# Attention output turned by one fp32r matmul per block, with its halves split by GpSimd and its sums moved by DMA

## What is computed

```python
q_pool = q.reshape(B, H, S // 2, 2, D).mean(axis=3)          # B=2, H=8, S=1152, D=64
scores = scale * np.matmul(q_pool, k.transpose(0, 1, 3, 2))
attn = np.exp(scores - np.max(scores, axis=-1, keepdims=True))
attn = attn / (np.sum(attn, axis=-1, keepdims=True) + 1e-09)
x = np.matmul(attn, v)      # then heads side by side: 1152 rows of 512
logits = x @ w_gate
noise_scale = np.log1p(np.exp(x @ w_noise))                  # both: 512 x 8
noisy_logits = logits + noise_scale * noise                  # picks two experts per row
...
```

## Time and profile before

| | |
|---|---|
| median of 3 runs | 845.34 us (844.6 to 846.09) |
| the profiled execution | 844.89 us, span of its trace 843.1 us |
| TensorE busy | 831.5 us (99%) |
| VectorE, ScalarE, GpSimd busy | 510.8, 418.7, 401.5 us |
| attention stage | up to about 305 us, of it 12 cycles of 18.0 us in the loop |
| granted TensorE clock | 1.000 over the span |

### The profile page before, as it was taken

How to read it: one execution, slowest core, us unless ns; L and a number is a source line. 1 busy time by engine, 2 the same in 40 slices (tenths; PEclk the granted TensorE clock), 3 DMA queues, 4 the chain that set the end, 5 groups by cost and what they waited for, 6 DMA issues and landing times.

```text
span 843.1 us, 15376 instructions
## 1 busy us (share of the span) xinstructions
PE 831.5 (99%) x4860; PEld 743.2 (88%) x4861; DVE 510.8 (61%) x1003; ACT 418.7 (50%) x770; POOL 401.5 (48%) x293
## 2 busy tenths in 40 slices
PE   7999999999999999999999999999999999999998
PEld 6999999999999898888887888888888999999997
DVE  7888888888888886322322223232286875576554
ACT  4777777777777774211211111121145765565554
POOL 8654455546887005548969959577432020000000
PEclk9999999999999999999999999999999999999999
DMA  5212111142241016887645635353445021000101
GB/s 131 71 45 82 43 42 42 42 148 80 92 151 69 1 57 222 299 302 231 234 145 187 199 137 199 131 192 131 143 124 164 1 75 38 2 0 1 38 1 37
DMA packets 51520, 91.27 MB, mean 108 GB/s; under 512 B 9376, under 2 KB 18592, under 8 KB 50976
## 3 DMA queue, kind: packets, MB, share of 16 engines
q1 hardware_dynamic: 40832, 67.26, 24.0%
q10 hardware_dynamic: 7296, 12.59, 4.5%
q0 software_dynamic: 3360, 11.01, 4.5%
HBM read 73.78 MB, written 17.06 MB: 108 GB/s over the span
## 4 chain that ended last, share of the span: by engine, by line
PE 94%; POOL 2%; DVE 1%; DMA 1%; issue 1%; ACT 1%; ACTq 0%; POOLq 0%; DVEq 0%
PE ps L1729 10%; PE ps L1731 10%; PE ps L1730 10%; PE ps L1536 5%; PE ps L1573 5%; PE ps L1589 5%; PE ps L1591 4%; PE ps L1590 4%; PE ps L1574 4%; PE ps L1885 4%; PE ps L1884 4%; PE ps L1883 4%; PE ps L1845 4%; PE ps L1843 4%; PE ps L1844 4%; PE ps L1527 3%
## 5 line engine op out<-in xcount | busy, mean ns | idle before, releaser
L652 POOL TENSOR_TENSOR W<-stage,W 128x2048 fp32r<-128x2048 f32 x32 | 147.4, 4606 | 2.6
L1067 DVE TENSOR_REDUCE mx<-ps 128x1 f32<-128x384 f32 x225 | 121.6, 551 | 9.7 <-PE ps L1536 8.2
L806 ACT ACTIVATE ph<-ps 128x576 fp32r<-128x576 f32 x144 | 93.9, 652 | 65.6 <-PE ps L1574 65.2
L1085 DVE TENSOR_TENSOR pl__81<-ps,ph 128x576 fp32r<-128x576 f32 x144 | 107.9, 750 | 14.0 <-ACT ps L813 13.8
L813 ACT ACTIVATE ps<-ps 128x576 f32<-128x576 f32 x144 | 93.5, 649 | 0.0
L1589 PE MATMUL ps<-ph,vs 128*65 128x288 f32 x288 | 86.2, 299 | 0.5 <-ACT ot L760 0.5
L897 ACT CAST hh<-ps 128x512 fp32r<-128x512 f32 x50 | 26.9, 590 | 120.0 <-PE ps L1768 120.0
L1591 PE MATMUL ps<-ph,vs 128*65 128x288 f32 x288 | 84.8, 294 | 0.0
L1590 PE MATMUL ps<-pl__81,vs 128*65 128x288 f32 x288 | 84.6, 294 | 0.0
L1573 PE MATMUL ps<-qat,kt 128*128 128x288 f32 x288 | 83.8, 306 | 0.6 <-ACT qbt L753 0.4
L1729 PE MATMUL ps<-W,xh 128*128 (+1 forms) x200 | 80.4, 402 | 1.0 <-POOL W L652 0.7
(11 more groups left out here) (238 smaller groups left out, 1965.8 us busy)
## 6 DMA issues: line engine op xcount, KB each, us to landing
stage<-in_moe_w_dram SPq DMA_DIRECT2D x32, 1024.0 KB
y_slots<-ys ACTq DMA_DIRECT2D x25, 256.0 KB
x_slots<-ring SPq DMA_DIRECT2D x22, 256.0 KB
xs<-x_slots ACTq DMA_DIRECT2D x22, 256.0 KB
kn<-in_k_dram SPq DMA_DIRECT2D x16, 288.0 KB, 3.4
vn<-in_v_dram SPq DMA_DIRECT2D x16, 288.0 KB, 2.8
stage<-in_moe_w_in_dram SPq DMA_DIRECT2D x4, 1024.0 KB
stage<-in_moe_w_out_dram SPq DMA_DIRECT2D x4, 1024.0 KB
```

What stands on the lines that cost most here:

```text
L652: pl.tensor_tensor(W[:, slot, 1, part], stage[:, j % 2, :], W[:, slot, 0, part].bitcast(F32), ALU.subtract).then_inc(w_ready, 1)
L1067: ve.tensor_reduce(mx3[:, i:i + 1], ps[:, bank_of(hh, ("m", i)), 0:PIECE], AX_X, ALU.max).then_inc(m_ev, 1)
L1085: ve.tensor_tensor(pl_[:, j % 3, :].rearrange("p (a n) -> p a n", a=2), ps[:, 2 * s_par(hh, j):2 * s_par(hh, j) + 2, 0:HQ], ph[:, j % 3, : ...
```

## The change

All turns but the last are done in fp32r with 128 rows. `ohl` holds the high halves of the head's output in rows 0 to 63 and the low halves in rows 64 to 127. GpSimd makes the high halves from `ot` and then, in place in `ot`, the low ones (`split_o`, three instructions). A DMA of SyncE's queue moves the low halves to rows 64 to 127 of `ohl`. `turner` has 128 rows and 96 columns a head: twice the identity one below the other, the high halves of the gate columns, and their low halves (zero below). So the logits come in two parts of 16 columns, which VectorE adds.

The sum of the weights no longer goes through the matmul: SyncE stores row 64 of `ot` to DRAM (scratch in `y_slots`) and loads it back with queries on partitions into `sums` (`turn_parts`: two loads of 4-byte pieces). `o_out` takes the reciprocal of `sums` ahead of the turn, copies the 32 logit columns of each block from PSUM to `both`, multiplies the rows into `x`, adds the halves in `both` and multiplies them into `shares`. The gate matrices are loaded once for both batches into `gates`, and GpSimd fills `turner` from them (`fill_turner`) where VectorE copied the identity before. Where readers of `shares` waited for `o_norm` they wait for `shared`. `turn_last` and `last_out` keep the fp32 form for head 15.

```diff
@@ VectorE
-            def o_out(p, hh, last=False):
+            def o_out(p, hh):
 
                 g = 2 * p + hh
+                dve.wait_ge(sums_in, 32 * (g + 1))
+                at_least(dve, shared, g)
+                ve.reciprocal(rinv[:, :], sums[:, :]).then_inc(rinv_done, 1)
                 dve.wait_ge(ot_done, g + 1)
-                at_least(dve, rinv_done, g)
-                at_least(dve, o_norm, g)
                 turned = ps[:, bank_of(hh, ("o", 0)), 0:QC * TURN].rearrange("p (c d) -> p c d", c=QC)
+                ve.tensor_copy(both[:, :, :], turned[:, :, D:TURN]).then_inc(both_done, 1)
+                dve.wait_ge(rinv_done, g + 1)
+                o_rows(g, turned)
+                dve.wait_ge(both_done, g + 1)
+                ve.tensor_tensor(both[:, :, 0:2 * E], both[:, :, 0:2 * E], both[:, :, 2 * E:4 * E], ALU.add
+                                 ).then_inc(halves_done, 1)
+                dve.wait_ge(halves_done, g + 1)
+                share = shares[:, bass.ds(g, 1), :, :].rearrange("p o c e -> p (o c) e")
+                ve.tensor_tensor(share, both[:, :, 0:2 * E], rinv[:, :].unsqueeze(2).to_broadcast([P, QC, 2 * E]), ALU.mult
+                                 ).then_inc(shared, 1)
...
@@ SyncE
+            def turn_parts(g, par):
+
+                row = y_slots[2 * par:2 * par + 2, :].rearrange("a n -> (a n)")
+                sp.wait_ge(ot_ev, g + 1)
+                sp.dma_start(row[0:SQ].unsqueeze(0), ot[D:D + 1, 0:SQ].bitcast(F32)).then_inc(row_out, 16)
...
+                sp.wait_ge(row_out, 16 * (g + 1))
+                sp.dma_start(sums[:, 0:QC - 1], row[0:4 * P].rearrange("(c p) -> p c", p=P),
+                             allow_slow_non_contiguous=True).then_inc(sums_in, 16)
+                sp.dma_start(sums[0:QTAIL, QC - 1:QC], row[4 * P:SQ].rearrange("(p o) -> p o", o=1)).then_inc(sums_in, 16)
+                sp.wait_ge(olo_done, g + 1)
+                sp.dma_start(ohl[D:P, 0:SQ].bitcast(F32), ot[0:D, 0:SQ].bitcast(F32)).then_inc(low_in, 16)
...
+                if not isinstance(m, int) or m >= 4:
+                    turn_parts(m - 4, par)
                 at_least(sp, v_ready, m - 1)
...
@@ GpSimd
+            def split_o(g):
+
+                pool.wait_ge(ot_ev, g + 1)
+                at_least(pool, ot_done, g)
+                pl.tensor_tensor(ohl[0:D, 0:EDGE], ot[0:D, 0:EDGE].bitcast(F32), zcol[0:D, :].to_broadcast([D, EDGE]), ALU.add)
+                pl.tensor_copy(ohl[0:D, EDGE:SQ], ot[0:D, EDGE:SQ].bitcast(F32)).then_inc(ohi_done, 1)
+                pool.wait_ge(ohi_done, g + 1)
+                pl.tensor_tensor(ot[0:D, 0:SQ], ot[0:D, 0:SQ].bitcast(F32), ohl[0:D, 0:SQ].bitcast(F32), ALU.subtract
+                                 ).then_inc(olo_done, 1)
...
                     copy_k(2 * p + par - 1, 1 - par)
+                    split_o(2 * p + par - 3)
                     split_v(p - 1 + par, 1 - par)
...
@@ ScalarE, o_move
-                at_least(act, ot_done, g)
+                at_least(act, low_in, 16 * g)
+                at_least(act, sums_in, 32 * g)
...
@@ TensorE
-            def turn_o(p, hh, halves=False):
+            def turn_o(p, hh):
+
                 g = 2 * p + hh
-                pe.wait_ge(half_ev if halves else ot_ev, 1 if halves else g + 1)
+                pe.wait_ge(low_in, 16 * (g + 1))
                 for c in range(QC):
...
-                    last = pe.matmul(ps[:, bank_of(hh, ("o", 0)), c * TURN:(c + 1) * TURN], ot[0:D + 1, c * P:(c + 1) * P],
+                    last = pe.matmul(ps[:, bank_of(hh, ("o", 0)), c * TURN:(c + 1) * TURN], ohl[:, c * P:(c + 1) * P],
                                      turner[:, bass.ds(g, 1), :].rearrange("p o n -> p (o n)"), start=True, stop=True)
                 last.then_inc(ot_done, 1)
```

More of the change, by code:

```diff
@@ L317, in build @@
         sine, at = place("sine", at, [P, 1])
+        sums, at = place("sums", at, [P, QC])
+        both, at = place("both", at, [P, QC, 4 * E])
+        gates, at = place("gates", at, [P, H, 2 * E])
+        turner_last, at = place("turner_last", at, [D + 1, TURN_LAST])
         assert at <= STG + 16384 + 6144, at
@@ L482, in _ @@
             load_head(0, 1)
-            for b in range(B):
-                for n, gate in enumerate((w_gate, w_noise)):
-                    sp.dma_start(turner[0:D, b * H:(b + 1) * H, D + 1 + n * E:D + 1 + (n + 1) * E],
+            for n, gate in enumerate((w_gate, w_noise)):
+                for half in range(2):
+                    sp.dma_start(gates[half * D:(half + 1) * D, :, n * E:(n + 1) * E],
                                  gate.rearrange("(h d) e -> d h e", d=D)).then_inc(gate_in, 16)
-            with sp.Fori(1, NHEAD // 2 - 2) as p:
+                sp.dma_start(turner_last[0:D, D + 1 + n * E:D + 1 + (n + 1) * E], gate[(H - 1) * D:H * D, :]
+                             ).then_inc(gate_in, 16)
+            for p in (1, 2):
+                load_head(p, 0)
+                load_head(p, 1)
+            with sp.Fori(3, NHEAD // 2 - 2) as p:
                 load_head(p, 0)
@@ L669, in _ @@
             split_v(0, 0)
-            with pool.Fori(1, NHEAD // 2 - 2) as p:
+            fill_turner()
+            for par in range(2):
+                split_kq(1, par)
+                copy_k(1 + par, 1 - par)
+                if par == 1:
+                    split_o(0)
+                split_v(par, 1 - par)
+            with pool.Fori(2, NHEAD // 2 - 2) as p:
                 for par in range(2):
@@ L1549, in low_queries, with turn_last @@
                 last.then_inc(qb_done, 1)
-            def turn_o(p, hh, halves=False):
+            def turn_o(p, hh):
                 g = 2 * p + hh
-                pe.wait_ge(half_ev if halves else ot_ev, 1 if halves else g + 1)
+                pe.wait_ge(low_in, 16 * (g + 1))
                 for c in range(QC):
-                    if halves and (c + 1) * P > HQ and c * P <= HQ:
-                        pe.wait_ge(ot_ev, g + 1)
-                    last = pe.matmul(ps[:, bank_of(hh, ("o", 0)), c * TURN:(c + 1) * TURN], ot[0:D + 1, c * P:(c + 1) * P],
+                    last = pe.matmul(ps[:, bank_of(hh, ("o", 0)), c * TURN:(c + 1) * TURN], ohl[:, c * P:(c + 1) * P],
                                      turner[:, bass.ds(g, 1), :].rearrange("p o n -> p (o n)"), start=True, stop=True)
+                last.then_inc(ot_done, 1)
+            def turn_last():
+                pe.wait_ge(half_ev, 1)
+                for c in range(QC):
+                    if (c + 1) * P > HQ and c * P <= HQ:
+                        pe.wait_ge(ot_ev, NHEAD)
+                    last = pe.matmul(ps[:, bank_of(1, ("o", 0)), c * TURN_LAST:(c + 1) * TURN_LAST],
+                                     ot[0:D + 1, c * P:(c + 1) * P].bitcast(F32), turner_last[:, :], start=True, stop=True)
                 last.then_inc(ot_done, 1)
```

91 lines of the change are left out of this document (62 added, 29 removed).

## The result

| | before | changed |
|---|---|---|
| median | 844.97 us (844.33 to 846.09, 4 runs) | 855.01 us (854.63 to 855.57, 4 runs) |
| span of the trace | 843.1 us | 852.8 us |
| ratio to before | | 1.0118 (95%: 1.0100 to 1.0135) |

The change costs 10.0 us. So the stated range holds the result only because it was stretched down to take in the case without a hold.

A forecast was written before the change was run, and what follows sets the result against it. TensorE is busy all 18.03 us of a cycle, paced by VectorE from the second maximum. Heads 0 to 11 +17.2, head 12 +0.1, head 13 -0.5, head 14 +0.2: +17.0 on 844.89, median 862.3 us, range 841 to 868.

The forecast's parts named there:

- the case without a hold: VectorE's two added instructions not held by GpSimd, 0.24 us each; 842.6 us, range 839.5 to 844.5, chance 0.20.
- the choice between the ends not held and held: VectorE's added sum of halves: 0.24 us, or held to the end of GpSimd's running instruction; held was taken.
- the start of the *second* maximum: VectorE's maximum of the second score piece, reckoned from the turn's start: 2.99 us before, taken as what counts.
- 1.40 and 1.47: Loss in us per head from the hold, by the second maximum: in mid-body and at the body's end.
- rival 1: No hold: odd heads 1 to 11 gain 0.34 us each, even heads 2 to 10 lose 0.09; 842.6 us, chance 0.20.
- at 1.8 us by its record: GpSimd's qa product, expected to be recorded at 1.8 us instead of 1.57 behind VectorE's held sum.
- 12 times 1.43: Heads 0 to 11: a loss of 1.43 us each from the hold, +17.2 us together.
- Head 12: Cycle behind head 12: GpSimd runs a short copy then, loss of 0.1 us.
- Head 13: Cycle behind head 13: no maxima in the next cycle, so TensorE's 0.54 us counts, -0.5 us.

The follow-up runs named there:

- v1: Changed kernel, but for heads 0 to 12 GpSimd adds the halves of the logits and multiplies the weights instead of VectorE; 839.16 us, ratio 0.9935.

## Why the prediction was right, and where it was off

**What held.** The chain: VectorE's two added instructions are the held kind, ask while GpSimd starts its next head, and TensorE pays by waiting for the maxima. They were to take about 0.6 and 1.5 us. The sum takes 0.48 to 0.65 for heads 0 to 7 and 0.26 for heads 8 to 11; the weights take 1.36 to 1.48 for all twelve. TensorE's idle time for VectorE was to be 2 us a cycle and is 1.17 before the third score piece, the cycle 19.45 and is 18.6 to 19.0. The low half by DMA has room, the turn takes 0.57 to 0.60 us for a forecast 0.54, and the choice between the ends not held and held, made by the earlier trace rows, was the right one: the same two instructions with one PSUM operand take 0.24 us.

**The handle was the wrong instruction.** The prediction reckoned the loss from the start of the *second* maximum. What TensorE waits for next is the end of the *first*, since the third score piece uses its bank. Over all kernels here, the start of the third score piece behind the start of the turn, and the cycle:

| kernel | first maximum starts | third piece | cycle | cycle less third piece |
|---|---|---|---|---|
| sums on GpSimd (v1) | 1.65 | 2.84 | 17.48 | 14.64 |
| before | 2.34 | 3.32 | 18.03 | 14.71 |
| v1, turn twice | 2.19 | 3.40 | 18.03 | 14.63 |
| before, two more with PSUM | 2.99 | 3.90 | 18.61 | 14.71 |
| changed, one operand in PSUM, middle | 2.22 | 3.13 | 17.74 | 14.61 |
| changed, GpSimd waits, middle | 2.22 | 2.84 | 17.51 | 14.67 |
| before, reciprocal and copy, middle | 3.43 | 4.37 | 19.08 | 14.71 |
| changed, with expert weights | 3.34 | 3.94 | 18.62 | 14.68 |
| changed, middle of the body | 3.57 | 4.17 | 18.86 | 14.69 |
| changed, end of the body | 3.65 | 4.25 | 18.97 | 14.72 |
| before, two more with SBUF | 4.91 | 5.85 | 20.55 | 14.70 |

A cycle is the third piece's start plus 14.6 to 14.7 us, whatever the kernel; reckoned from the second maximum, the rest varies more, from 14.8 (changed) to 15.0 (before). The cycles at a lower clock and the one behind head 12 (14.05 to 14.26) are not in the table. The third piece starts 0.6 behind the first maximum's start, or 0.70 behind the second piece, whichever is later; where VectorE's added work also keeps the bank of the turn (the kernels with two more instructions, and the one with an operand in PSUM in the middle of the body), it is the second piece that comes late, and the third 0.8 behind it. In the kernel before the third piece had 0.38 us to spare over the first maximum (2.34 plus 0.6 against 3.32). The prediction's own times, a first maximum at 3.87 and 3.94, give 1.15 and 1.22 by this handle, not 1.40 and 1.47: 3.0 of the 7.3 us of error. It also mis-sized rival 1: without a hold the middle cycles gain 0.5 (17.52 in the kernel in which GpSimd waits), not 0.34.

**A held instruction of 80 elements delays GpSimd by nothing.** The prediction let GpSimd's product start only when VectorE's sum was done, 0.24 later, at 1.8 us by its record. The cast starts at 148.02 and the product at 148.64, 0.62 apart, as in the earlier trace rows (143.57 and 144.19), and the product takes 1.56. The prediction had its rule from the earlier trace rows, where GpSimd's instruction behind a held copy of 1040 elements took 1.59 us for the usual 1.14; no such delay shows behind 80 elements, and no run here varies the size in between. Nor is there a gap to the first maximum, which starts 0.02 behind GpSimd's end. So the first maximum came 0.30 us earlier than forecast, 3.5 us over 12 heads.

**Heads 8 to 11 were not looked at apart.** In the cycles with expert weights GpSimd is busy until shortly before the turn and takes up its next head sooner. In the timeline of the changed kernel it starts 0.32 us behind the turn of head 9, after a wait of 0.56, where it starts 0.55 behind that of head 5, after 7.45:

```profile
222.34 0.87 POOL L658 TENSOR_TENSOR qp<-qn 128x320 f32<-128x320 f32 x1 [0.56 <-PE ps L1616]
...
223.16 0.66 POOL L659 CAST ks<-kn 128x576 fp32r<-128x576 f32 x1
...
223.66 0.26 DVE L1179 TENSOR_TENSOR both<-both 128x80 f32<-128x80 f32 x1
...
223.79 1.55 POOL L660 TENSOR_TENSOR qa<-qn 128x640 fp32r<-128x640 f32 x1
...
224.07 1.37 DVE L1183 TENSOR_TENSOR shares<-both,rinv 128x80 f32 x1
```

The cast has only 0.16 us left when the sum is asked for, so the sum loses next to nothing, and the product, with all behind it, ends 0.23 sooner. The trace of before had the same shift (0.24 us against 0.47 and 0.56), so the step that failed was "12 times 1.43" from two cycles taken for twelve. It is worth 1.0 us (third piece at 3.94 and 3.96 instead of 4.17 and 4.25), and with the two terms above it makes 7.5 of the 7.7 us by which heads 0 to 11 were over-forecast (17.2 against 9.5).

**Head 12 was held too.** Its sum of halves takes 0.70 us, held by GpSimd's cast of K, which ends 2.24 us behind the turn; the cycle loses 0.3, where 0.1 was forecast.

**Head 13 was given the wrong sign.** Its 0.5 us were to be TensorE's gain in full. The turn did gain it, and the held gap took 0.8 back, 0.25 in all. The prediction asked which of *VectorE's new* instructions GpSimd would hold, and not which *old* ones GpSimd's new instructions would.

## What to carry over

When work moves to GpSimd, or VectorE gets an instruction with both operands in SBUF or a copy from SBUF to SBUF, lay the two engines' timelines over each other at that place: such an instruction of VectorE, even of 5 elements, ends when GpSimd's running one ends, and if GpSimd's next has already started when it is asked for, it waits for the whole of that one. It is cured by leaving one operand in PSUM, by letting GpSimd do it, or by a wait that starts GpSimd later where it has room. And before a delay is turned into time, find the instruction of the bounding engine that waits next and its spare time, here one bank further up than the prediction looked.

## What was not expected of the hardware

A waiting VectorE instruction of 80 elements did not delay the GpSimd instruction behind the one that it waited for, where a copy of 1040 had: casts and products start 0.62 us apart with and without it. VectorE's ends 0.09 to 0.10 us after GpSimd's for products and sums of 80 elements, 0.06 for the copy of 80, 0.03 for the gap of 5. GpSimd answers the same semaphore of TensorE sooner when it has hardly waited: 0.32 us behind the start of the turn after a wait of 0.56, 0.55 after one of 7.45; why, no run here shows. A reciprocal costs 0.65 us for 80 elements and 0.18 for 5, while a product of 80 takes 0.24.
